# Attention: pooled q turned one block a step in a ring bank, its high part on ScalarE and its low part on GpSimd

## The reference

```python
def _attn_ref(q, k, v):                      # 4 batches, 8 heads, 1152 rows, 64 columns
    B, H, S, D = q.shape
    factor = 2
    scale = 1.0 / np.sqrt(D)
    q_pool = q.reshape(B, H, S // factor, factor, D).mean(axis=3)      # 576 pooled rows
    scores = scale * np.matmul(q_pool, k.transpose(0, 1, 3, 2))        # 576 x 1152
    scores = scores - np.max(scores, axis=-1, keepdims=True)
    attn = np.exp(scores)
    attn = attn / (np.sum(attn, axis=-1, keepdims=True) + 1e-09)
    return np.matmul(attn, v).astype(np.float32)
```

## Time and profile before

| | before |
|---|---|
| median of three runs | 1211.71 us |
| the profiled execution, its own time | 1212.04 us |
| its span | 1210.3 us |
| attention (PE's last row of it starts at) | 588.0 us |
| one pair in the loop | 35.66 us |

### The profile page before, as it was taken

One profiled execution on the slowest core, in us unless ns is written; L12 is line 12 of the kernel. 1 busy time (PEld: TensorE's weight loads), 2 busy tenths in 40 slices (PEclk: granted clock), 3 DMA queues, 4 the chain that ended last, 5 costly groups with the idle time before them and its releaser, 6 DMA issues.

```text
span 1210.3 us, 23735 instructions
## 1 busy us (share of the span) xinstructions
PE 1125.0 (93%) x7465; PEld 1033.2 (85%) x7466; DVE 764.4 (63%) x1457; ACT 568.7 (47%) x1044; POOL 538.8 (45%) x597
## 2 busy tenths in 40 slices
PE   6999999999999999999689899999938999799997
PEld 5999999999999999999679798989926787677785
DVE  4888888889889888889633254444623523452532
ACT  4666666666666676666242333324304421432311
POOL 6777777777787777775210001010224400440400
PEclk9999999999999999999789999999958999899999
DMA  5545442354543345543230104020235521531110
GB/s 189 143 145 155 138 138 100 100 155 145 155 136 123 90 127 146 155 116 97 85 94 1 40 1 147 1 74 1 75 110 212 176 81 38 220 110 44 35 41 25
DMA packets 68110, 125.94 MB, mean 104 GB/s; under 512 B 8238, under 2 KB 19630, under 8 KB 68080
## 3 DMA queue, kind: packets, MB, share of 16 engines
q1 hardware_dynamic: 38720, 53.01, 14.2%
q10 hardware_dynamic: 23376, 52.59, 13.9%
q0 software_dynamic: 5984, 19.95, 4.8%
HBM read 69.25 MB, written 57.33 MB: 105 GB/s over the span
## 4 chain that ended last, share of the span: by engine, by line
PE 39%; DVE 4%; DMA 3%; ACT 2%; issue 2%; POOL 0%; DVEq 0%; ACTq 0%; SPq 0%; POOLq 0%
PE second_ps L1610 10%; PE first_ps L1602 8%; PE wide L913 7%; PE tall L913 5%; PE tall L982 2%; PE smalls L982 2%; PE ht_ps L1594 1%; DMA w_raw<-moe_w 1%; DMA rows_in<-sorted_tokens 1%; PE xt_ps L1587 1%; DVE spatial_l L1268 1%; DVE val L1264 1%; ACT spatial_h L1132 1%; DVE w_l L1739 0%; PE smalls L1039 0%
## 5 line engine op out<-in xcount | busy, mean ns | idle before, releaser
L639 DVE TENSOR_SCALAR_CACHE_REDUCE probs<-scores 128x1152 f32<-128x1152 f32 x144 | 195.5, 1358 | 61.3 <-PE scores L484 60.3
L484 PE MATMUL scores<-k_t,q_t 128*128 128x384 f32 x960 | 202.3, 348 | 1.3 <-DVE probs L639 1.3
L583 ACT ACTIVATE probs<-probs,neg_max 128x1152 f32<-128x1152 f32 x144 | 181.7, 1262 | 0.0
L614 ACT CAST pt_h<-ring 128x384 fp32r<-128x384 f32 x288 | 138.6, 481 | 73.9 <-PE ring L491 68.0
L507 PE MATMUL acc<-pt_h,v_parts 128*128 128x256 f32 (+1 forms) x576 | 169.1, 316 | 0.6 <-DVE pt_l L705 0.6
L491 PE MATMUL ring<-consts,probs 128*128 128x128 f32 x1296 | 165.4, 273 | 0.7 <-DVE pt_l L705 0.7
L484 PEld LDWEIGHTS scores<-k_t,q_t 128*128 128x128 f32 x960 | 161.2, 189 | 2.2 <-DVE probs L639 2.1
L507 PE MATMUL acc<-pt_l,v_parts 128*128 128x256 f32 (+1 forms) x576 | 157.2, 295 | 0.0
L340 POOL TENSOR_TENSOR pt_l<-mid,pt_h 128x384 fp32r<-128x384 f32 x144 | 145.6, 1011 | 12.0
L491 PEld LDWEIGHTS ring<-consts,probs 128*128 128x128 f32 x1296 | 146.4, 142 | 2.4 <-DVE pt_l L705 1.8
L705 DVE TENSOR_TENSOR pt_l<-ring,pt_h 128x384 fp32r<-128x384 f32 x288 | 145.8, 548 | 0.0
(11 more groups left out here) (226 smaller groups left out, 2542.8 us busy)
## 6 DMA issues: line engine op xcount, KB each, us to landing
sorted_tokens<-pad_row ACTq DMA_DIRECT2D x16, 2570.0 KB, 12.6
x_and_u<-moe_w POOLq DMA_DIRECT2D x10, 1024.0 KB, 6.1
k_nat<-k SPq DMA_DIRECT2D x32, 288.0 KB, 2.7
v_nat<-v SPq DMA_DIRECT2D x32, 288.0 KB, 4.5
q_nat<-q SPq DMA_DIRECT2D x32, 256.0 KB, 2.9
w_raw<-moe_w ACTq DMA_DIRECT2D x3, 2048.0 KB, 12.5
rows_in<-sorted_tokens SPq DMA_DIRECT2D x23, 257.0 KB, 2.6
x_heads<-x_pair SPq DMA_DIRECT2D x16, 256.0 KB, 4.2
```

Of the source, the lines that this page charges most:

```text
L484: mm = nc.tensor.matmul(scores[:, c, 0:CK], q_t[par][:, side, t * P:(t + 1) * P], k_t[par][:, c * CK:(c + 1) * CK], start=(i == 0), stop=( ...
L583: nc.scalar.activation(probs[n % 3][:], probs[n % 3][:], ACT.Exp, bias=neg_max[:, n % 3:n % 3 + 1], scale=-1.0, accum_out=row_sum[:, n:n + ...
L614: nc.scalar.copy(pt_h[:, 3 * c:3 * c + 3, n * P:(n + 1) * P], ring[c][:, 0:CK].rearrange("p (i r) -> p i r", i=3)).then_inc(s["high_done"], 1)
L639: nc.vector.tensor_scalar(probs[n % 3][:], scores[:, :, 0:CK], -0.5 * DH ** -0.5, None, ALU.mult, ALU.min, accum_out=neg_max[:, n % 3:n % ...
```

## The change

q is no longer split before it is turned. GpSimd adds the two rows of q and writes the sum twice, side by side (`sum_q`, one addition into `q_sums`). In each step the middle ring bank gets a fourth transpose, `turn_q`, one block of the doubled sum (columns 384 to 511). DVE's copy to `mid` takes all 512 columns. From `mid` ACT writes the high part (`q_high`) after its two casts and before the exponential, and GpSimd writes the low part (`q_low`) after the tile's own low part. The block turned in step n is tile n+5 (AHEAD_Q = 5), whose scores are taken in step n+3. The two heads' shared block is one block, with the other head's columns held at zero in `q_t`, which now holds both heads.

The q prep jobs go away; k's six jobs all stand in slot 1 and all go to SBUF on ACT. The addition of 1e-9 goes from DVE to GpSimd (`add_eps`). The start is written anew: the first four blocks of q are turned together, their low part is DVE's, and the first scores wait for head A alone.

```diff
-    q_nat = [sb(f"q_nat{i}", [P, QT, 2, DH]) for i in range(2)]
-    q_sums = [sb(f"q_sum{i}", [P, QT, DH]) for i in range(2)]
-    q_parts = [sb(f"q_parts{i}", [P, QT, 3, DH], F32R) for i in range(2)]
-    q_t = [sb(f"q_t{i}", [P, 2, QT * P], F32R) for i in range(2)]
-    mid = [sb(f"mid{i}", [P, CK]) for i in range(3)]
+    q_nat = [sb(f"q_nat{i}", [P, SHARED + i, 2, DH]) for i in range(2)]
+    q_sums = sb("q_sums", [P, NT, 2, DH])
+    q_t = sb("q_t", [P, 2, NT + 1, P], F32R)
+    mid = [sb(f"mid{i}", [P, CK + P]) for i in range(3)]
...
     EXTRAS = {
-        0: (("prep", 1, 3), ("prep", 1, 4)),
-        1: (("fold", 2), ("prep", 1, 5)),
+        0: (None, ("prep", 1, 2)),
+        1: (("fold", 2), None),
         2: (None, ("fold", 3)),
-        3: (("prep", 0, 0), ("prep", 0, 1)),
-        4: (("prep", 0, 2), ("prep", 0, 3)),
-        5: (("prep", 0, 4), ("prep", 0, 5)),
+        3: (None, ("prep", 0, 0)),
+        4: (None, ("prep", 0, 1)),
+        5: (None, ("prep", 0, 2)),
         6: (("fold", 0), None),
-        7: (("prep", 1, 0), ("prep", 1, 1)),
-        8: (("fold", 1), ("prep", 1, 2)),
+        7: (None, ("prep", 1, 0)),
+        8: (("fold", 1), ("prep", 1, 1)),
     }
...
+            def sum_q(par, j):
+
+                pool.wait_ge(q_loaded[par], (16 + 32 * par) * (j + 1))
+                pool.sem_inc(s["pool_go"], 1)
+                tiles = slice(par * SHARED, par * SHARED + SHARED + par)
+                a, b = (q_nat[par][:, 0:SHARED + par, r].unsqueeze(2).to_broadcast([P, SHARED + par, 2, DH])
+                        for r in range(2))
+                nc.gpsimd.tensor_tensor(q_sums[:, tiles], a, b, ALU.add).then_inc(s["split_done"], 1)
+
+            def q_low(tile, n):
+
+                i = (n + AHEAD_Q) % NT
+                pool.wait_ge(s["q_high"], tile + AHEAD_Q + 1)
+                pool.sem_inc(s["pool_go"], 1)
+                low(q_piece(1, i), q_turn_of(mid[n % 3][:, CK:CK + P], i), q_piece(0, i), s["q_low"])
...
                 high(pt_h[:, 3:6, cols], src, s["mid_step"])
+                for g in range(len(FOLDS)):
+                    if FOLDS[g][-1] == n:
+                        add_eps(g)
                 pool.wait_ge(s["mid_step"], highs)
                 low(pt_l[:, 3:6, cols], src, pt_h[:, 3:6, cols], s["mid_split"])
+                if has_piece(n, after):
+                    q_low(tile, n)
...
-            def turn(n, c):
+            def turn(n, c, piece):
                 for i in range(3):
                     mm = nc.tensor.transpose(ring[c][:, i * P:(i + 1) * P],
                                              probs[n % 3][:, c, i * P:(i + 1) * P], ident)
+                if piece:
+                    mm = turn_q(ring[c][:, CK:CK + P], (n + AHEAD_Q) % NT)
                 mm.then_inc(s["turned"], 1)
...
                 if n + 2 < NT or after:
                     pe.wait_ge(s["neg_done"], tile + 2)
+                    pe.wait_ge(s["q_low"], tile + 3)
...
+            def q_high(tile, n):
+
+                i = (n + AHEAD_Q) % NT
+                act.wait_ge(s["mid_done"], tile + 1)
+                nc.scalar.copy(q_piece(0, i), q_turn_of(mid[n % 3][:, CK:CK + P], i)).then_inc(s["q_high"], 1)
...
                                    ).then_inc(s["high_done"], 1)
+                if has_piece(n, after):
+                    q_high(tile, n)
                 if n + 2 < NT or after:
                     exp(tile + 2, (n + 2) % NT)
...
-                nc.vector.tensor_scalar(row_eps[:, cols], row_sum[:, cols], 1e-9, None, ALU.add
-                                        ).then_inc(s["sum_step"], 1)
-                dve.wait_ge(s["sum_step"], 8 * pair + 2 * g + 1)
-                nc.vector.reciprocal(row_inv[:, cols], row_eps[:, cols]).then_inc(s["sum_step"], 1)
+                dve.wait_ge(s["eps_done"], 4 * pair + g + 1)
+                nc.vector.reciprocal(row_inv[:, cols], row_eps[:, cols]).then_inc(s["inv_done"], 1)
...
-                nc.vector.tensor_copy(mid[n % 3][:], ring[1][:, 0:CK]).then_inc(s["mid_done"], 1)
+                width = CK + P if has_piece(n, after) else CK
+                nc.vector.tensor_copy(mid[n % 3][:, 0:width], ring[1][:, 0:width]).then_inc(s["mid_done"], 1)
```

## The result

| | before | after |
|---|---|---|
| median | 1211.78 us | 1198.07 us |
| single runs | 1211.71 to 1214.4 | 1195.06 to 1199.46 |
| the profiled execution's span | 1210.3 us | 1196.6 us |
| first turns of a tile on PE | 21.07 | 21.86 |
| one pair in the loop | 35.66 | 34.54 |

The ratio is 0.9878, 95% interval 0.9855 to 0.9902. Forecast was 1193 (1186.5 to 1203): faster, as forecast, by 13.7 us instead of 18.9.

A forecast was written before the change was run, and what follows sets the result against it. PE's gapless work was taken to bound the kernel. Fifteen pairs at 1.14 us (17.1), the last pair 0.4 and the start 1.4 sum to 18.9 us off 1212.04; forecast 1193 us, range 1186.5 to 1203.

The forecast's parts named there:

- PE's work laid end to end sets the pair: Attention loop: PE busy 35.52 of a pair's 35.66 us, so a transpose taken off shortens the pair by its spacing.
- PE's sum, -1.44: PE per pair: q jobs -2.02, exponentials' turns +0.90, moved k jobs +0.12, stalls -0.44 us, before any new wait.
- the slot-0 jobs: Transpose jobs ahead of a step's scores: four q transposes priced at 0.35 us, three k at 0.24.
- The stalls, -0.44: PE's waits for DVE to free bank `misc`: 0.19 us gained in step 3, 0.25 in step 8, per pair.
- The deadline in step 5: PE's product at kt 3 needs tile 4's low part from POOL; PE would wait 0.3 us once a pair.
- The slot-1 jobs: Transpose jobs behind a step's scores: should start 1.15 us after the scores everywhere, a sign the forecast holds.
- ACT costs the path nothing: ACT's `q_high` delays the exponential some 0.7 us, covered by the 8 us ACT idles.
- Rival 2: ACT's hand-over delays casts, DVE's low parts and PE's turns: 0.1 us in each of nine steps, 1206 us; chance 0.09.
- rival 1: No wait of PE for POOL in step 5: 1188.3 us; chance 0.16.
- rival 4: DVE's or the transfers' rhythm keeps the pair at 35.66 us, the gain taken up elsewhere: 1211 us; chance 0.03.
- The start, 1.4: Before the loop: one addition replaces the first head's q split, so PE's first transposes start at 7.4, 1.4 us earlier.
- What follows attention shifts as a block: The time behind attention is untouched by the change and was taken to keep its length.

The follow-up runs named there:

- the transpose twice: Changed kernel with each step's q block turned twice into the same place: 1207.89 us in one run, pair 35.09.
- the k jobs: Kernel with head B's low part of k behind tile 4, five k jobs moved from behind the scores to ahead of them: 1189.44 us, pair 33.90.
- the late low part of k: Changed kernel with GpSimd's low part of k of head B placed behind tile 4's parts instead of before them: 1185.29 us, ratio 0.9785.
- the high part twice: Kernel with head B's low part of k behind tile 4, ACT writing each q block's high part twice: 1190.07 us, pair 34.05.
- the filled starts: Twenty idle transposes in PE's start gaps: on the changed kernel 1193.75 us; with head B's low part of k also behind tile 4, 1183.53 and 1183.74.
- the second trace: The changed kernel run again, unaltered, on the chip of the next three runs: 1195.46 us, ratio 0.9859.
- the low part done twice: Changed kernel with GpSimd's low part of each q block done twice, once into an unread tile: 1217.63 us in one run.

## Why the prediction was right, and where it was off

- **That PE's work laid end to end sets the pair: right.** Every edit that took or gave PE work showed in the pair at its spacing (the transpose twice, the k jobs, the late low part of k with PE busy 33.84 of 33.84 us).
- **PE's sum, -1.44: too small, 1.82.** The term that was mis-sized is the slot-0 jobs. They were priced by the distance to the next group alone. The five score groups that no longer follow transposes take 1.05 instead of 1.15, five times 0.10, as the k jobs ahead of the scores confirm. Against it, ten transposes take 1.01 where 1.00 was taken, and a fold behind the scores of the shared tile 0.42 instead of 0.39.
- **The stalls, -0.44: right in kind.** Of the 0.25 in step 8, done alone, came 0.32: 0.27 at the scores, and 0.05 at the k job behind them, which the prediction had booked among the jobs that move. The 0.19 of step 3 is gone too (1.34 before, 1.05 after).
- **The deadline in step 5: right place, 0.3 should have been 0.7.** Counted from the start of step 2's turns, PE would ask 11.52 us later where it was 12.53: 1.01 earlier and not 0.70, mainly because three of those score groups stand before it. (The prediction named the end of the middle bank's turns as its start, but its four q turns are the count from the start of step 2's turns, as here.) POOL comes 0.79 later where 0.84 was taken; inside that the addition to the row sums takes 0.22 and a gap of 0.08 where 0.10 was taken, and `q_low` at 0.42 from start to start gives 0.16 back. From the end of POOL's low part to PE's product pass 0.06, and the interruption itself costs 0.10 in the next product. So 0.29 + 0.31 - 0.05 + 0.06 + 0.10 = 0.71.
- The last two errors nearly cancel: 1.82 - 0.70 = 1.12 against 1.44 - 0.30 = 1.14. That the pair came out right to 0.02 us was luck, two errors of 0.4 us that met, and only the run that removed the wait showed it. The slot-1 jobs, said to start 1.15 us after the scores everywhere, start 1.05 after them in five steps, which was the sign.
- **ACT costs the path nothing: true of this change**, but with less room than the idle 8 us suggested, as the high part twice shows. Rival 2 fell, as did rival 1 with the wait in step 5 and rival 4 with the shorter pair.
- **The start, 1.4: the step that failed.** It was worked out with the clock as in the trace of before. The chain itself was right: the first transposes start at 7.47 where 7.4 was forecast, and with score products of 1.3 us the gain is 1.44. But PE now idles 1.9 to 2.0 us before the first scores, and in seven of nine traces some groups of score products of the start took 2.26 to 2.29 us instead of 1.3. In the profiled one the clock column reads 0.50 beside them, and it paid 2.2 us. That the idle time slows the products behind it is likely from the filled starts, and not shown beyond their three traces.
- **What follows attention shifts as a block: only roughly.** It took 622.3 us before and 623.9 after, but between 619.8 and 626.6 in the traces of this study, the kernel with the old start and only the two-column addition moved among them at 626.5. The code there is the same; between the two first traces the difference came in pieces of 0.4 to 0.9 us, back and forth, at several places, and 0.5 in the transfer between the stages. At one of these places, where 0.7 us are lost within 1 us of work, the low clock lasted longer: 0.50 in the kernel after (655.6 to 657.6 us) and 0.70 at the same place before (671.0 to 673.0). Why an execution gets more or less of this stays open; no run was made on it. It is 1.6 of the missing 5.2 us; the start is 2.2; the rest, 1.4, lies in the pairs (0.3) and in the first and last steps of attention, of which the turns of step 0, also at the low level in that trace, are 0.7 (1.97 us from them to the next scores, 1.29 in the second trace).

## What to carry to other kernels

Price an instruction in a gapless queue by what its neighbours take with and without it, not by the distance to the next start alone; and price a wait the same way, since the idle time that a profile shows can leave out a third of it (0.45 us in the view here, 0.71 by the starts). When work is added to an engine with idle time, look for the one consumer that comes soonest after its densest stretch, and put whatever has a later deadline behind it: moving one 1.43 us instruction of each pair gave 10 us. A tiny VectorE instruction on SBUF alone beside a busy GpSimd can last as long as GpSimd's instruction (0.98 us for two columns beside 1.01 here), so such small ones are the first to move.

## What the runs showed of the hardware that was not expected

- PE's speed in the first 25 us differs from execution to execution of the same instructions: the same milestone fell between 19.57 and 22.92 us. With twenty idle transposes in the gaps it fell between 19.74 and 20.01, in three traces. That the filling, and not chance, keeps the score products at 1.3 to 1.6 us is likely from that but rests on three traces.
- Six products of 384 columns start 1.05 us before the next group behind products of the same kind, and 1.13 to 1.15 behind fp32 transposes.
- The column of the granted clock can read 1.00 where six score products take 2.26 to 2.29 us, nearly twice their usual 1.3, so durations are the safer sign.
- With the low part done twice, the granted clock fell to 0.50 behind PE's wait of 1.8 us in four of fifteen pairs, which then took 1.6 us more, and stayed at 1.00 behind the same wait in the other eleven.
- DVE's reciprocal of two or three columns, also on SBUF alone, was never held: 153 to 169 ns in the changed kernel, though 63 of the 64 began while a GpSimd instruction was running, where DVE's two-column addition of the kernel before was held in most cases (158 to 992 ns, median 973; 62 of the 64 began while a GpSimd instruction was running and ended 0.01 to 0.03 us behind it).
